# The 160 middle steps of a step-scheduled kernel: written out, or as a loop of five passes over 32 steps

## The reference

```python
    x_pad = np.concatenate([np.zeros((B, pad, D), dtype=np.float32), x], axis=1)
    idx = np.arange(S)[:, None] + np.arange(K)[None, :]
    x_unf = x_pad[:, idx, :].reshape(B, S, K, H, group)
    out = np.einsum('hk,bskhg->bshg', w, x_unf)
...
    h = x @ w_in
    relu6 = np.clip(h + 3.0, 0.0, 6.0)
    g = h * relu6 / 6.0
    return (g @ w_out).astype(np.float32)
...
    h = x @ w_in
    h2 = h * h
    h3 = h2 * h
    P = a[0] + a[1] * h + a[2] * h2 + a[3] * h3
    Q = 1.0 + np.abs(b[0]) * np.abs(h) + np.abs(b[1]) * h2
    g = P / (Q + 1e-06)
    return (g @ w_out).astype(np.float32)
```

## Time and the profile before

| | |
|---|---|
| median of three runs | 1255.71 us (1255.02 to 1256.53) |
| the profiled execution's own time | 1255.71 us |
| its span, first to last instruction | 1253.9 us |
| outside the span | 1.8 us |
| instructions in the trace | 18222 |
| TensorE matmul, busy | 1194.4 us |
| VectorE, busy | 1170.2 us |
| ScalarE, busy | 1168.9 us |
| GpSimd, busy | 1080.4 us |
| granted TensorE clock, mean | 0.988 |

### The profile page before, as it was taken

How to read it: one execution, slowest core, us unless ns; L and a number is a source line. 1 busy time by engine, 2 the same in 40 slices (tenths; PEclk the granted TensorE clock), 3 DMA queues, 4 the chain that set the end, 5 groups by cost and what they waited for, 6 DMA issues and landing times.

```text
span 1253.9 us, 18222 instructions
## 1 busy us (share of the span) xinstructions
PE 1194.4 (95%) x5120; PEld 963.1 (77%) x5120; DVE 1170.2 (93%) x1784; ACT 1168.9 (93%) x2223; POOL 1080.4 (86%) x828
## 2 busy tenths in 40 slices
PE   4989999999999999999999999999999999999766
PEld 3767778888788888888788887888878887888554
DVE  6779999999999999999999999999999999998797
ACT  4779999999999999999999999999999999999896
POOL 3759898998989899998989989998999989888565
PEclk8999999999999999999999999999999999999899
DMA  4310000000000000010000100000000000000000
GB/s 123 125 39 10 1 22 1 17 14 1 22 1 22 10 7 16 1 31 1 22 1 1 30 1 23 1 22 10 1 22 1 22 1 14 1 1 13 1 14 13
DMA packets 10005, 21.17 MB, mean 17 GB/s; under 512 B 1712, under 2 KB 1712, under 8 KB 9904
## 3 DMA queue, kind: packets, MB, share of 16 engines
q1 hardware_dynamic: 9760, 19.55, 5.3%
q10 hardware_dynamic: 144, 0.46, 0.1%
HBM read 13.72 MB, written 6.29 MB: 16 GB/s over the span
## 4 chain that ended last, share of the span: by engine, by line
PE 79%; DVE 11%; issue 5%; ACT 5%; POOL 0%; DMA 0%; SPq 0%; ACTq 0%; DVEq 0%; POOLq 0%
PE h L236 39%; PE y0b_acc L253 4%; PE y0a_acc L248 4%; PE y0b_acc L254 4%; PE y0a_acc L250 4%; PE y0a_acc L249 4%; PE y1a_acc L248 4%; PE y1b_acc L254 4%; PE y1a_acc L249 4%; PE y1b_acc L253 4%; PE y1a_acc L250 4%; DVE num L365 2%; DVE h L397 2%; DVE g L404 1%; ACT h L387 1%
## 5 line engine op out<-in xcount | busy, mean ns | idle before, releaser
L377 POOL TENSOR_TENSOR den<-den,sqr 128x512 f32<-128x512 f32 x256 | 377.4, 1474 | 124.7 <-ACT den L354 123.8
L415 POOL TENSOR_TENSOR g_lo<-g,g_hi 128x512 fp32r<-128x512 f32 x256 | 336.2, 1313 | 1.9 <-ACT g_hi L421 1.9
L341 POOL TENSOR_TENSOR g_lo<-r,g_hi 128x512 fp32r<-128x512 f32 x234 | 307.5, 1314 | 0.0
L370 DVE SCALAR_TENSOR_TENSOR num<-num,coef,h 128x512 f32<-128x512 f32 x256 | 191.5, 748 | 9.1
L397 DVE SCALAR_TENSOR_TENSOR h<-num,coef,h 128x512 f32<-128x512 f32 x256 | 191.8, 749 | 0.0
L392 DVE SCALAR_TENSOR_TENSOR den<-den,h 128x512 f32<-128x512 f32 x256 | 174.5, 682 | 17.5 <-ACT h L387 15.3
L381 ACT ACTIVATE rsq<-den 128x512 f32<-128x512 f32 x256 | 165.3, 646 | 25.8 <-POOL den L377 24.9
L365 DVE TENSOR_TENSOR num<-num,h 128x512 f32<-128x512 f32 x256 | 175.1, 684 | 12.4 <-ACT num L348 4.8
L348 ACT ACTIVATE num<-h,coef 128x512 f32<-128x512 f32 x256 | 182.2, 712 | 0.0
L404 DVE SCALAR_TENSOR_TENSOR g<-den,h 128x512 f32<-128x512 f32 x256 | 174.3, 681 | 0.7
L421 ACT ACTIVATE g_hi<-g 128x512 fp32r<-128x512 f32 x256 | 168.7, 659 | 3.2 <-DVE g L404 1.6
(11 more groups left out here) (93 smaller groups left out, 2886.6 us busy)
## 6 DMA issues: line engine op xcount, KB each, us to landing
stage_w<-w_pack SPq DMA_DIRECT2D x15, 448.0 KB, 3.3
raw_a<-x_a SPq DMA_DIRECT2D x16, 259.0 KB, 3.4
out<-y_a SPq DMA_DIRECT2D x16, 256.0 KB, 2.7
raw_b<-x_b SPq DMA_DIRECT2D x16, 129.5 KB, 2.7
out<-y_b SPq DMA_DIRECT2D x16, 128.0 KB, 2.4
stage_w<-w_pack ACTq DMA_DIRECT2D x1, 448.0 KB, 3.5
tap_a<-taps SPq DMA_DIRECT2D x1, 3.5 KB, 2.9
tap_b<-taps SPq DMA_DIRECT2D x1, 3.5 KB, 4.0
```

Source lines behind the costliest of these rows:

```text
L341: eng.tensor_tensor(g1_lo[q.off % 2][:, :], gated(q)[:, :], f32(g1_hi[q.off % 2][:, :]), ALU.subtract).then_inc(S["g1lo"], 1)
L370: eng.scalar_tensor_tensor(out=n, in0=n, scalar=a1, in1=h2_of(q), op0=ALU.add, op1=ALU.mult).then_inc(S["num1"], 1)
L377: eng.tensor_tensor(d, d, sqr[q.off % 2][:, :], ALU.add).then_inc(S["den_sum"], 1)
L415: eng.tensor_tensor(g2_lo[q.off % 2][:, :], g2[q.off % 2][:, :], f32(g2_hi[q.off % 2][:, :]), ALU.subtract).then_inc(S["g2lo"], 1)
```

## The change

The step loop of `run` is split in three. Steps 0 to 63 are written out as before, with the loading of the weights among them. Steps 64 to 223 become a loop in the hardware program, on every engine: its body is 32 steps written out, and it is passed N_LOOP = (256 - 32 - 64) / 32 = 5 times. Each engine has its own counter and its own branch at the end of the body; there is no barrier among the engines in it. Steps 224 to 300 are written out as before. Inside the loop every step is `Step(p, i, STEPS)`, so that each wait is against `i * per + off` in a register instead of a constant, and so is each transfer's column. The stages, their order, their buffers and the semaphores they wait for are the same.

```diff
         LAST = NT + SUM2 + 4
+        P_START = 2 * STEPS
+        N_LOOP = (NT - STEPS - P_START) // STEPS
+        P_END = P_START + N_LOOP * STEPS
+        assert P_START > SUM2 + 1 and P_END <= NT + PAIR_AHEAD
+
...
-            for p in range(LAST):
-                emit(eng, plan if p < NT else late(plan), Step(p))
+            for p in range(P_START):
+                emit(eng, plan, Step(p))
                 for c in range(1, n_layers * n_chunks):
                     if weights and p == weight_step(c) - early:
                         weights(c)
+            with eng.Fori(0, N_LOOP) as i:
+                for p in range(P_START, P_START + STEPS):
+                    emit(eng, plan, Step(p, i, STEPS))
+            for p in range(P_END, LAST):
+                emit(eng, plan if p < NT else late(plan), Step(p))
```

## The result

The changed kernel took 1261.81 us (median of six runs, 1260.88 to 1262.99), the one before 1255.55 us (six runs, 1253.31 to 1256.53): a ratio of 1.0052, 95% interval 1.0039 to 1.0065. The loop costs 6.3 us. The forecast was 1266.1 in a range of 1257 to 1284, slower with 0.84.

What follows compares the result with a forecast made beforehand. TensorE was taken to set the pace in the looped steps. Taken branches 7.2 us plus register values 3.2 us made 10.4 us on 1255.71 us: 1266.1 us, range 1257 to 1284.

Steps and rivals of the forecast that it cites:

- What bounds the kernel: Steps 64 to 224: TensorE busy 732.89 of 735.03 us sets the pace; at most 2.1 us to win.
- Taken branches: Four back edges per engine: fetch 3.0 us less DVE's cover 1.2, so 1.8 us each, 7.2 us in all.
- The branches themselves: Four compare-and-branches at the loop's end, an estimated 0.4 us, lying inside the fetch's gap.
- The head must be fetched again, on every engine.: At each back edge every engine's sequencer waits for the loop head's code, 3.0 us; TensorE's share in the sum is nothing.
- Gaps overlap rather than add: Engines reach each edge within 4.2 us of each other, so only DVE's gap, the longest at 1.8 us, counts.
- the 4 to 7 of the rival: At the edges engines wait for one another's fetches in turn: 4 to 7 us an edge, 1272 to 1284 us; chance 0.17.
- Register values: Waits in the loop need one or two register operations each: 0.02 us a step, 3.2 us.
- The rival with registers in every step: Register operations cost 0.05 to 0.10 us in every loop step, 8 to 16 us: 1271 to 1279 us; chance 0.16.
- The clock: Rival: TensorE's granted clock falls after the edges, some 3.5 us an edge, 1280 us; chance 0.05.
- Hidden edges: Rival: at the edges, cover plus the gate's 1.2 us lead hides the fetch, 1255.7 us, at most 2 more; chance 0.16.

Runs made afterwards that it cites:

- the kernel with the edges apart: The changed kernel with ScalarE's loop begun 16 steps earlier, at step 48, the other engines' at step 64: 1266.16 us, ratio 1.0098 to the kernel before.
- the first hinted loop: The changed kernel with hint_back_edge=True on each engine's loop, same five passes of 32 steps: 1256.89 us, ratio 1.0020 to the kernel before.
- the kernel with two loops: The changed kernel with its loop cut into two hinted loops, of two and three passes over 32 steps: 1261.77 us, ratio 1.0054 to the kernel before.

## Why the prediction was right, point by point

**What bounds the kernel.** Right. TensorE sets the pace, and what stops DVE or ACT for longer than their margin stops it.

**Taken branches.** Right in mechanism, place and size. The fetch was taken as 3.0 us; it was 2.8 to 3.0 on DVE and 2.4 to 2.7 on ACT. That this came so close is in part luck: no row had the fetch, and 3.0 was picked between 0.5 and 4.0 us by likeness with transfers of other sizes. The cover on DVE was taken as 1.2 us and its gap as 1.8; the gap was 1.84 at step 128 and 1.7 on average. TensorE's loss was taken as the whole gap, 7.2 us for four edges; it was 7.15 in the profiled execution, and by the medians the whole change cost 6.3. The hint, which takes away the fetch alone, takes the passes back to 147.0. The branches themselves, an estimated 0.4 us for four, were about 0.2: 63 ns each on DVE, 45 on ACT. By the rule of the Trainium skill (Runtime: NRT & Kernel Launch, Instruction fetch mechanics) a taken branch waits for a fetch when its target is not in the two-block window. On DVE, ACT and POOL the runs agree if a block is the packet seen here, 128 instructions: bodies of 364, 576 and 359 instructions were fetched and one of 193 was not. With the Trainium skill's block of 256 instructions, those of 359 and 364 would have been in the window. The time that it doesn't give is 2.4 to 3.0 us on these engines, and 3.9 on TensorE.

**"The head must be fetched again, on every engine."** Wrong for two of them. TensorE's body of some 1350 instructions and POOL's of some 190 were at hand; twice as long, both were fetched. For TensorE that is what the Trainium skill's 2048 instructions (same page and section) would make, and the runs with the loop of 32 and of 64 steps lie on either side of it; the window of two blocks, 512 instructions by its figures, would not have held 1350. The prediction had expected more packets on queue 8 as well; there were half as many. It changed nothing in the sum, in which neither had a share, and the kernel with the loop on TensorE, GpSimd and SyncE alone shows that they have none.

**Gaps overlap rather than add.** Right, and shown from both sides: alone the two engines cost 5.8 and 6.3 us, together 6.3, apart 12.1. In the kernel with the edges apart the gaps do add, but at 12.1 / 4 = 3.0 us for a pair of edges, not at the 4 to 7 of the rival.

**Register values.** This term was mis-sized: 3.2 us were taken, none is there. The first pass in the loop takes 147.06 us, and all five of the first hinted loop 146.9 to 147.0. The count of operations was off as well: 33 to 66 a step were allowed for, and the trace has 1274 more instructions in 160 steps, 8 a step. (The size of DVE's body was undercounted too: nine waits for six stages leave 3 x 32 = 96 second and third waits, not some 70.) The rival with registers in every step falls with it. Without the term the sum is 1262.9 us, against 1261.81 measured.

**The clock.** It stayed at full grant in the whole stretch (1.00 in the windows). That rival fell.

**Hidden edges.** The cover would have had to be 3 us on DVE and ACT. On TensorE (4.1 us of queued work) and on POOL it was nearly there: with the body of 64 steps they hid all but some 0.2 and 0.4 us of their own fetches. On DVE and ACT it was 1.2 us, and the 1.2 us by which the gate is early at the edge did not save the rest, as the prediction had argued.

## What to carry to other kernels

As far as this kernel shows, a loop costs, at each taken branch, a fetch of the code at its head less what the engine has queued, if the body is longer than the engine keeps; work it out engine by engine, since the one with shallow queues pays and TensorE may not. Keep the edges of the engines at the same place in the schedule, so that their gaps overlap, or loop only on engines that don't pay. Hints pay with many passes and few exits; count the exits too.

## What the runs showed of the hardware that was not expected

GpSimd's body of 32 steps was passed again 0.3 us after the branch, with no fetch; at 64 steps the same branch was followed by 2.6 us. TensorE's branch took 0.21 us when its body was at hand, 3.88 when it wasn't, 0.39 with the hint. A fetch on DVE took 2.8 us from branch to next instruction, of which its packet was 0.5. Waits against a register's value, at eight more sequencer instructions a step over all engines, left a schedule with 3% of slack unchanged. Hinted loops ran their passes at full pace (146.8 to 147.0 us; one of 147.5 in the kernel with two loops), but the 16 steps behind its exit took 1.6 to 3.3 us more.
